# A linear-attention and two-MoE-block kernel: attention in steps of 64 tokens instead of 128, and operands moved to multiples of 512 bytes

## The reference, cut to what matters

```python
for t in range(S):                       # B, H, S, D = 4, 8, 768, 48
    cur = einsum('bhd,bhe->bhde', u[None] * kt, vt)
    y[:, :, t] = einsum('bhd,bhde->bhe', rt, state + cur)
    state = w[None, :, :, None] * state + einsum('bhd,bhe->bhde', kt, vt)
x = y as (3072, 384)
h = maximum(maximum(x @ w1, x @ w2), x @ w3)        # d_ff 768
x = h @ w_out
xn = x / sqrt(mean(x * x) + 1e-6) * rms_g           # second block, d_ff 1536
out = (silu(xn @ w_gate) * (xn @ w_val)) @ w_out2
```

## Time and profile before

| | us |
|---|---|
| median of 3 runs (lowest, highest) | 926.01 (924.24, 926.2) |
| profiled execution | 925.77 |
| its span, first to last instruction | 923.8 |
| PE busy in the span | 884.6 (96%) |
| PE weight loads (PEld) | 797.9 (86%) |
| DVE, ACT, POOL busy | 429.2, 318.7, 156.5 |

### The profile page before, as it was taken

The page is one execution under the profiler, slowest core; times in us unless marked ns, Lnnn a source line. Parts: engine busy times, 40 slices in busy tenths (PEclk is TensorE's granted clock), DMA queues, the critical chain, the costliest instruction groups (busy, mean ns, idle before and its releaser), DMA issues.

```text
span 923.8 us, 13898 instructions
## 1 busy us (share of the span) xinstructions
PE 884.6 (96%) x4776; PEld 797.9 (86%) x4776; DVE 429.2 (46%) x985; ACT 318.7 (35%) x716; POOL 156.5 (17%) x197
## 2 busy tenths in 40 slices
PE   3679999999999999999989999999999999999998
PEld 3579999999999999999978888888888888888886
DVE  8977565546555564643542432252252342243221
ACT  2453333334333332433344432323233233233112
POOL 5542223232222323200332400000000000000000
PEclk9779999999999999999999999999999999999999
DMA  7263213121311312102212100000000000000000
GB/s 239 89 216 109 62 55 108 63 61 55 111 57 54 114 54 60 54 6 68 86 52 69 35 3 32 1 1 35 1 1 34 0 0 34 0 0 25 10 0 35
DMA packets 45142, 48.28 MB, mean 52 GB/s; under 512 B 3504, under 2 KB 36656, under 8 KB 45104
## 3 DMA queue, kind: packets, MB, share of 16 engines
q1 hardware_dynamic: 45104, 47.79, 16.6%
HBM read 41.88 MB, written 4.72 MB: 50 GB/s over the span
## 4 chain that ended last, share of the span: by engine, by line
PE 89%; DVE 7%; issue 3%; ACT 1%; DMA 0%; DVEq 0%; ACTq 0%
PE h_b L415 16%; PE h_b L417 15%; PE h_b L416 15%; PE y_b L417 8%; PE y_b L415 8%; PE y_b L416 8%; PE a_b L401 4%; PE s_b L386 4%; PE s_b L416 3%; PE s_b L417 3%; PE s_b L415 3%; DVE kd L782 2%; PE a_b L405 2%; PE a_b L409 1%; DVE A L792 1%
## 5 line engine op out<-in xcount | busy, mean ns | idle before, releaser
L415 PE MATMUL h_b<-xh,Wh 128*128 128x384 f32 (+1 forms) x594 | 216.3, 364 | 6.1 <-DVE xl L816 4.8
L417 PE MATMUL h_b<-xh,Wl 128*128 128x384 f32 (+1 forms) x594 | 208.7, 351 | 0.0
L416 PE MATMUL h_b<-xl,Wh 128*128 128x384 f32 (+1 forms) x594 | 208.5, 351 | 0.0
L417 PE MATMUL y_b<-hh,Wl 128*128 128x512 f32 (+1 forms) x360 | 132.7, 369 | 0.0
L415 PE MATMUL y_b<-hh,Wh 128*128 128x512 f32 (+1 forms) x360 | 132.4, 368 | 0.2 <-DVE hl L991 0.2
L416 PE MATMUL y_b<-hl,Wh 128*128 128x512 f32 (+1 forms) x360 | 132.5, 368 | 0.0
L415 PEld LDWEIGHTS h_b<-xh,Wh 128*128 128x128 f32 x594 | 112.2, 189 | 13.0 <-issue 5.0
L416 PEld LDWEIGHTS h_b<-xl,Wh 128*128 128x128 f32 x594 | 112.3, 189 | 6.4
L417 PEld LDWEIGHTS h_b<-xh,Wl 128*128 128x128 f32 x594 | 111.9, 188 | 6.3
L718 ACT CAST hh<-hB 128x512 fp32r<-128x512 f32 x72 | 44.7, 621 | 165.2 <-DVE hB L986 163.0
L328 POOL TENSOR_TENSOR rd<-rbuf,PR 112x128 f32<-112x128 f32 x96 | 45.6, 475 | 271.9 <-PE a_b L409 237.3
(11 more groups left out here) (124 smaller groups left out, 1298.7 us busy)
## 6 DMA issues: line engine op xcount, KB each, us to landing
vbuf<-in_v SPq DMA_DIRECT2D x24, 320.0 KB, 4.1
kbuf<-in_kT SPq DMA_DIRECT2D x24, 256.0 KB, 3.6
rbuf<-in_rT SPq DMA_DIRECT2D x24, 256.0 KB, 3.7
rnbuf<-in_r SPq DMA_DIRECT2D x24, 192.0 KB, 2.4
knbuf<-in_k SPq DMA_DIRECT2D x24, 192.0 KB, 2.5
x<-in_wA SPq DMA_DIRECT2D x6, 768.0 KB, 7.6
out_t<-xraw SPq DMA_DIRECT2D x5, 768.0 KB, 3.8
wst<-in_gv SPq DMA_DIRECT2D x6, 384.0 KB, 3.1
```

What stands on the lines that cost most here:

```text
L415: nc.tensor.matmul(bank[:, 0:n], hi, xhi, start=first, stop=False)
L416: nc.tensor.matmul(bank[:, 0:n], hi, xlo, start=False, stop=False)
L417: return nc.tensor.matmul(bank[:, 0:n], lo, xhi, start=False, stop=last)
```

## The change

Attention's products are taken in two halves u of 64 tokens (SUB = 64) inside the same chunk of 128. `kd`, `vv` (a new copy of v spread over 112 columns, zero elsewhere) and `kn` are laid out so that one matmul serves both heads of a pair for one half: head 0's 64 tokens on the first 64 rows of the contraction, head 1's on the other 64. The state is updated after each half, so a slot is cut into `front` (half 0) and `back` (half 1); `back` of slot k comes one slot later in PE's order, behind the scores of slot k + 2 and ahead of the `front` of slot k + 1, and waits for the middle update of `T`. A number takes 13 places in PE's order instead of 12. ScalarE spreads v (`spread_v`, two copies a chunk). The rings of `rd`, `kd`, `A` have 3 places. The decay tables have 64 columns instead of 128. The memory layout of r, k, v in HBM is permuted accordingly; v's rows have 384 elements instead of 640. `gcol`, `eps` and a gap of 320 bytes stand ahead of `Wh`, so that `Wh` and all that is listed under addresses above, Xh and the others too, begin at a multiple of 512 bytes.

```diff
-SLOTS = (("w1", "out"), ("w1", "w2", "out"), ("w1", "out"), ("w1", "w2", "out"), ("w1", "out"), ())
+SLOTS = (("w1", "w2", "out"), ("w1", "out"), ("w1", "w2", "out"), ("w1", "out"), ("w1", "w2", "out"), ())
...
+        gcol = sb(ctx, "gcol", [P, KC])
+        eps = sb(ctx, "eps", [P, 1])
+
+        sb(ctx, "gap", [P, 80])
         Wh = sb(ctx, "Wh", [P, F1 * W1F], F32R)
...
             def scale_k(i, par, j):
...
+                for u in range(2):
+                    own = slice(u * NPAIR, (u + 1) * NPAIR)
+                    last = nc.gpsimd.tensor_tensor(
+                        by_head(kn[:, n % 2, own, :]),
+                        knbuf[:, j, :].rearrange("t (x e) -> t x e", e=D)[:, own, None, :].broadcast_to([P, NPAIR, 2, D]),
+                        by_head(PKn[:, :, :]), ALU.mult)
+                last.then_inc(kn_scaled, 1)
...
             def prep_r(i, par, k, first=False, following=None, ahead=False):
-                wait(pool, y_ready, number(i, par) * Q + k - 3)
+                wait(pool, y_ready, number(i, par) * Q + k - RING + 1)
...
             def scores(i, par, k, bank, ring=1):
-                for half in range(2):
-                    last = nc.tensor.matmul(bank[:, half * C:(half + 1) * C], kd[0:R, k % 4, half, :], rd[0:R, k % 4, :],
+                for u in range(2):
+                    last = nc.tensor.matmul(bank[:, u * SUB:(u + 1) * SUB], kd[0:R, k % RING, u, :], rd[0:R, k % RING, u, :],
                                             start=True, stop=True)
...
+            def attend(i, par, k, bank, u):
...
+                last = nc.tensor.matmul(bank[0:R, at:at + SUB], vv[:, n % 2, x, :], A[:, k % RING, u, :],
+                                        start=True, stop=(n == 0 and u == 0))
+                if n > 0 or u > 0:
+                    last = nc.tensor.matmul(bank[0:R, at:at + SUB], T[0:R, pair, 0:R], rd[0:R, k % RING, u, :],
+                                            start=False, stop=True)
+                if n < UPD or u == 0:
+                    last = nc.tensor.matmul(bank[0:R, NEW + u * D:NEW + (u + 1) * D], kn[:, n % 2, x, 0:R], vbuf[:, j, x, :],
+                                            start=True, stop=True)
+                return last
...
+            def back(i, par, k, bank, ring=1):
+
+                q = number(i, par) * Q + k
+                if ring == 1:
+                    wait(pe, y_evac, q)
+                pe.wait_ge(mid_state, q + 1)
+                attend(i, par, k, bank, 1).then_inc(y_ready, 1)
...
             def group(g, par, ai=None, apar=None, first=False):
-                            attend(ai, apar, slot, a_b)
+                            if slot > 0:
+                                back(ai, apar, slot - 1, a_b)
+                            if slot < Q:
+                                front(ai, apar, slot, a_b)
...
             def take_y(i, par, k, bank):
+                if k + 1 < Q:
+                    act.wait_ge(mid_state, number(i, par) * Q + k + 2)
...
             def slot_work(i, par, k, a_bank, before_bank, next_s_bank, following=None):
...
+                if k > 0 and GC * par + (k - 1) // NPAIR < UPD:
+                    sum_state(i, par, k - 1, before_bank, 1, shared=before_bank is a_bank)
+                if k < Q:
+                    sum_state(i, par, k, a_bank, 0)
```

More of the change, by code:

```diff
@@ L33 @@
 C = 128
+SUB = C // 2
+MID = SUB // 2
+RING = 3
 NPAIR = H // 2
@@ L253, in _ @@
             sp.dma_start(wcol[:], w).then_inc(cols_loaded, 16)
-            sp.dma_start(urow[:], u.partition_broadcast(P)).then_inc(u_loaded, 16)
+            for half in range(2):
+                sp.dma_start(urow[half * HB:(half + 1) * HB], u[half].partition_broadcast(HB)).then_inc(u_loaded, 16)
             for j in range(GC):
@@ L397, in attend @@
                 pe.wait_ge(masked, q + 1)
-                vv = vbuf[:, j, pair, :]
-                for half in range(2):
-                    nc.tensor.matmul(bank[0:R, 0:C], vv[:, half * D:half * D + R], A[:, k % 4, half, :],
-                                     start=(half == 0), stop=(half == 1 and n == 0))
                 if n > 0:
                     pe.wait_ge(state_ready, updates(i, n - 1, k))
-                    last = nc.tensor.matmul(bank[0:R, 0:C], T[0:R, pair, 0:R], rd[0:R, k % 4, :], start=False, stop=True)
@@ L406, in attend @@
-                if n < UPD:
-                    pe.wait_ge(kn_scaled, UPD * i + n + 1)
-                    heads = bass.AP(vv.tensor, vv.offset, [list(vv.ap[0]), [R, 2], [1, D]])
-                    last = nc.tensor.matmul(bank[0:R, C:C + 2 * D], kn[:, n % 2, pair, 0:R], heads,
-                                            start=True, stop=True)
-                last.then_inc(y_ready, 1)
+                attend(i, par, k, bank, 0).then_inc(half_ready, 1)
+            def back(i, par, k, bank, ring=1):
+                q = number(i, par) * Q + k
+                if ring == 1:
+                    wait(pe, y_evac, q)
+                pe.wait_ge(mid_state, q + 1)
+                attend(i, par, k, bank, 1).then_inc(y_ready, 1)
@@ L876, in group @@
                         sum_current(nexti, nextpar, 0)
-                        for k in range(NPAIR):
+                        for k in range(RING):
                             prep(nexti, nextpar, k)
@@ L890, in then @@
                 dve.wait_ge(powers, steps[0])
-            nc.vector.memset(PK[:, :, HB - 1:HB], 1.0)
-            nc.vector.memset(PR[:, :, HB:HB + 1], 1.0)
+            nc.vector.memset(PK[:, :, MID - 1:MID], 1.0)
+            nc.vector.memset(PR[:, :, MID:MID + 1], 1.0)
+            nc.vector.memset(vv[:], 0.0)
+            dve.wait_ge(consts_ready, 1)
+            for half in range(2):
+                own = slice(half * SUB, (half + 1) * SUB)
+                nc.vector.tensor_copy(mask[own, :], upper[own, own])
+                last = nc.vector.tensor_copy(diag[own, :], ident[own, own])
```

228 lines of the change are left out of this document (133 added, 95 removed).

## The result

The changed kernel takes 980.37 us (median of 4 runs, 978.24 to 983.4) against 925.91 for the kernel before: 1.0599 times as long, with a 95% interval from 1.0573 to 1.0625. Forecast were 954 us and a range from 908 to 962. The profiled execution of after is its fastest, 978.2. By stages, from the first records of each in both traces: the first number ends at 67.27 us instead of 54.64 (+12.6); from the first block's start to the first Xh matmul 460.9 us pass instead of 415.5 (+45.4); from there to the end 448.4 instead of 453.7 (-5.4).

A forecast was written before the change was run, and what follows sets the result against it. PE's issue bounds both blocks, DVE only attention's first number. From 925.8 us, slots +26.3, waits +3, first number +4 and addresses -5.4 gave 953.7, say 954 us; range 908 to 962.

The forecast's parts named there:

- The slots, +26.3: Attention slots beside the first block: weight loads outlast short streams, a full slot takes 1.62 us instead of 1.31; +26.3 us.
- The addresses, -5.4: MoE matmuls with weights from Xh: back in step with xh, each drops from 20 to 13.3 ns extra; -5.4 us.
- Rival A: MoE matmuls: distance to 512 bytes is what costs, so aligned addresses remove most of the 13.3 ns; 915 us, chance 0.35.
- the 13.3 ns of all others: Full-clock float32r MoE matmuls already in step: extra 13.3 ns each, seemingly a price of the load; no change taken.
- The new waits, +3 with bounds 0 and +15: Seven numbers beside the first block: back waits for T's middle update and the output copy; +3 us, ACT's additions nothing.
- The first number, +4 with bounds 0 and +10: First number of attention: DVE sets the pace, and added updates and scale_k outweigh savings; +4 us.
- The DMAs, 0: Loads of v: smaller rows take 128 KB a chunk (24%) off DMAs that hide already; 0 us.
- Rival B: Chain through DVE and ACT binds, late by 0.4 us at each short gap, 20 us on top; 970 us, chance 0.08.
- the 49 short gaps: Shortest gaps before the next back, 2.0 us each; Rival B had DVE late by 0.4 us in each.
- Rival C: Attention slots: loads hide behind short streams, making attention worth -40 us; 885 us, chance 0.07.

The follow-up runs named there:

- the two mended kernels: Changed kernel, and kernel before with new addresses, each with ScalarE's number-start work half a group earlier and GpSimd's two subtractions in the first block: 964.9 and 917.01 us.

## Why the prediction was right in part and too low

Direction and main mechanism held; two terms of the sum were too small, and for both the step behind them was wrong. Against the profiled execution of after, 978.2 where the sum said 953.7, 24.5 us are missing.

- **The slots, +26.3.** Right: 1.63 us by the rows. By distances between ends, full slots without a wait have a median of 1.63 and a mean of 1.65, where before has 1.32 and 1.33. The two runs that changed moving columns alone and the one that halved the weight columns show that the loads make it.
- **The addresses, -5.4.** Right, and shown alone (6.0 by medians, 5.4 in the second block of the profiles). Rival A is out: the time is the same at 0 and at 192 bytes past a multiple of 512. That the 13.3 ns of all others look like a price of the load beside them was a guess that halved loads did not bear out.
- **The new waits, +3 with bounds 0 and +15.** This step failed. The first block grew by 45.4, of which 84 x 0.318 = 26.7 are slots; 18.7 are waits and what follows them. I had looked at the gap between `back` and the output's copy and put "ACT's two spread copies a chunk and the halved diagonals and placements" at nothing, since ACT is busy 141 of 385 us. That share is an average: at a number's start these instructions stand in ScalarE's queue behind the last split of the group before, nothing covers them, and PE's scores wait. It is 8.8 us more than before at six starts, and the clock's fall behind three of them. Moving them gave 10 to 12 us back, so the queue is shown for all starts but one: 2.5 us at that one stayed, behind VectorE and with an open cause. What is left besides are nine places where `back` comes 0.34 us late, for ACT's copy behind VectorE's sum L838 (the place that the forecast had named), some 3 us together, and the first group, 3.0 us beyond its slots, in which matmuls are 0.320 us apart until 75 us (before: until 57 us). For these I have rows but no run.
- **The first number, +4 with bounds 0 and +10.** This step failed too, with 12.6. "Here DVE sets the pace" was read from busy shares of before. In after PE has 14 to 16 records a slot at the lower clock, 3.11 us, and sets the pace itself from 24 to 49 us; this is shown by the slots that grew by exactly the extra matmul. Six such slots make 4.9 us of the difference between the two mended kernels. The longer chain also puts VectorE's last third for Wl beside GpSimd's doubled scale_k and both subtractions, where it is held for 8.53 us, and moving the subtractions starts the first block 7.6 us earlier. But little of the growth is in this, some 2 us at most: before paid for the same subtractions with two held preparations of kd, and with the move in both kernels 12.3 us stay. The 7.4 us beside those six slots, 3.9 ahead of them and 3.5 behind, have no run that explains them.
- **The DMAs, 0.** The size of this term was right, its reading was not: 128 KB are 11% of a chunk's 1216 KB of loads, not 24%, and the share of 0.24 is that of the first block; in the first number it is 0.36.
- **Rival B** had the right place, the chain through DVE and ACT, but the wrong point in it: not the 49 short gaps, but the starts of a number. **Rival C** fell with the slots.

The range ended at 962 because I closed the bounds of the waits (+15) and of the first number (+10) against each other; with both at their ends the sum would have been 972, still short of the 978.2 measured.

The Trainium skill ("SBUF — State Buffer", section Who interferes with whom) says that a VectorE instruction with two SBUF inputs contends with a GpSimd instruction that reads SBUF and that the loser blocks for that instruction. The rows agree on who is held (kd and Wl, not T, which has one input in PSUM), but not on how long: 4.17 and 8.53 us go over four GpSimd instructions in a row. Held by one instruction alone, the same subtraction took 1.35 us.

## What to carry to other kernels

Splitting a matmul with short streams buys nothing where its weight load is as long as the stream: count records times their load, not columns. Where instructions are added to an engine with much idle time, look at the place in its queue, above all where one loop's work ends and the next one's begins; behind three of six such waits PE's clock fell as well. Before a stall is named as the cause of a difference, look whether the other kernel has it too: here the mend had to go into both. And keep weights and moving operand in step; 0, 128 and 192 bytes past a multiple of 512 gave the same 226.7 ns.

## What the runs showed of the hardware that I had not expected

- A VectorE operation with two inputs in SBUF stayed held over a whole run of four GpSimd instructions, also where short ones had taken the place of long ones: 3.86 us for an instruction of some 0.3.
- A change between weights of 128 and of 64 columns costs PE 0.14 us each way. The Trainium skill ("TensorEngine Tiling (Array Packing)", section Key Properties) says that a change of tiling mode drains TensorE; the two steps of the run agree, if these shapes count as two modes.
- PE at work from 24 to 49 us, with 0.2 us of pause at most before 49, stayed at 1.2 GHz. In after the clock's column reads 1.00 there, and the distances (0.213 and 0.187 us a record against 0.111 and 0.098) tell it; in the run with one extra matmul a slot the same distances stand beside 0.50. In the run with three a slot and 24 ahead it was at 2.4 GHz for most of that time (0.92 on the mean from 24 to 66 us).
- Operands out of step by 64 or 128 bytes cost a float32r matmul of 512 columns some 6 ns, by 192 or 256 only 2 to 4 on the mean.
